# Moving the inner rows of a mixture of experts through DRAM and turning them on VectorE, with the second layer two tiles behind the first

## The chip, the cores and the metric

One core of one Trainium2 chip. The metric is the device time of one execution in microseconds. Three runs of the kernel before gave 1191.72, 1190.87 and 1191.61 us; the median is 1191.61 us.

## The reference, cut to what matters

Three stages run one after the other: a small attention, a dense two-layer network, and a mixture of experts. The change touches the last alone:

```python
N, D, E, F = 4352, 512, 8, 1024      # rows, width, experts, inner width
e_idx = np.argmax(x @ w_gate, axis=1)
for e in range(E):
    mask = e_idx == e
    h  = np.maximum(x[mask] @ w1[e], 0.0)     # first layer, 512 -> 1024
    ye = h @ w2[e]                            # second layer, 1024 -> 512
    out[mask] = gate_w[mask, None] * eom[mask, e, None] * ye
```

Everything is fp32. Each fp32 product is made of three fp32r products: both operands are split into a high part (a copy rounded to fp32r) and a low part (what is left), and hi*hi, hi*lo and lo*hi are summed.

## The kernel before, in words

The first two stages end at about 700 us of the profile and are the same in both kernels. They leave each row in a DRAM table, `buckets`, sorted by expert, and VectorE works out a small `table` of numbers from the counts: for each tile of 128 rows the bucket row at which it starts (T_ROW), the ordinal of its expert (T_ORD), whether the weights of the next expert are split during it (T_SPLIT) and those of the expert after that loaded (T_LOAD), and which of two weight slots is used. With the inputs drawn, the experts that occur get 4, 5, 13, 5, 1, 5 and 5 tiles, in this order: 38 tiles, numbered 0 to 37, with new experts at tiles 4, 9, 22, 27, 28 and 33. T_SPLIT is set at the third tile of an expert, or at its last if it has fewer: at tiles 2, 6, 11, 24, 27 and 30.

Every engine runs its own program over the tiles, in order, and waits on semaphores (`wait`, `wait_ge`). `loops` (L434) writes out the first PEEL = 3 tiles, then a hardware loop of four tiles per turn, then the tiles that may be empty, each inside an If. `entry` (L430) reads a number of the table into a register of the engine; the profile shows it as TENSOR_LOAD at L432.

TensorE (`body`, L919) does for tile t:

- `first(t)` (L877): 24 matmuls of 128x128x512 in two halves of 12, from the turned rows `xg_t` and the split weights `we` into the two banks of `h_ps`;
- `second(t-1)` (L903): 24 matmuls from `act_t` and `we` into `y_ps`;
- `transpose_hid(t)` (L893): 8 transposes (matmuls against `ident`) of `expert_hid`, the rows after the relu, into two other banks of `y_ps`. They wait for act_ready0 and act_ready1.

ScalarE (`body`, L1092): relu of the first half of tile t (L1097), high part of the next tile's rows (`rows_hi`, L1084), three table reads, if T_SPLIT the high parts of the next w1 in four pieces (L1059), the high parts of the turned inner rows (L1119, from PSUM), and if T_SPLIT those of w2. VectorE (`body`, L1506) does the relu of the second half (L1510), the low part of the next rows (L1380), low parts of the weights (L471), the gate scaling of the tile before (`put_out`, L1494), the low parts of the inner rows (L1529), and the 32x32 block transposes of the rows of tile t+2 (`turn_rows`, L1384). The rows are turned by VectorE too: SyncE loads them in four strips of 32 partitions so that block transposes are enough.

SyncE (`body`, L585) loads the rows of tile t+3 (four DMAs of 64 KB, L559, and one small one for the gates, L562), and if T_LOAD the raw w1 and w2 of the expert after next (2 MB each, L568 and L571), each as soon as its buffer has been split. GpSimd stores the finished rows with an indirect DMA (L668).

## Time and profile before

| | |
|---|---|
| median of 3 runs | 1191.61 us |
| the profiled execution | 1192.12 us |
| its span, first to last instruction | 1190.4 us (1.7 us lie around it) |
| granted TensorE clock, mean | 0.990 |
| TensorE matmul busy | 1162.4 us (98%) |
| VectorE busy | 620.1 us (52%) |
| ScalarE busy | 440.4 us (37%) |
| DMA | 91.46 MB, mean 77 GB/s |

Busy time counts tensor instructions only: an engine's table reads, branches, waits and DMA issues are not in it. Matmuls are pipelined, so a matmul of about 390 ns starts every 230 ns. The chain of waits follows the end of the span back to what released each piece; "ACTq" and "DVEq" there are the sequencers of ScalarE and VectorE, "SPq" that of SyncE.

### The profile page before, as it was taken

What the parts mean: (1) busy time and instruction counts of PE and PEld (TensorE: products, weight loads), DVE (VectorE), ACT (ScalarE), POOL (GpSimd) and SP (SyncE); (2) the same over time, 40 slices, a digit from 0 to 9 for tenths busy, and PEclk for the clock granted to TensorE, in tenths of its full rate; (3) what the DMA queues carried; (4) which work ended last, traced back from release to release, by engine and by line L of the source; (5) the groups of instructions that cost most, each with busy time, mean ns of one, the idle gap of its engine ahead of it and who ended that gap; (6) DMA issues with size and microseconds to landing.
All of it is one profiled execution on the core that took longest, in us unless ns stands there. A gap on an engine that the chain in (4) does not pass through costs nothing.

```text
span 1190.4 us, 21176 instructions
## 1 busy us (share of the span) xinstructions
PE 1162.4 (98%) x6662; PEld 916.9 (77%) x6663; DVE 620.1 (52%) x1208; ACT 440.4 (37%) x742; POOL 81.4 (7%) x96
## 2 busy tenths in 40 slices
PE   9999999999999999999999978999999999999995
PEld 7777777777777777777778966888888888878874
DVE  6675655646646546465554464654543334566331
ACT  4454444444344434444543342341412122344110
POOL 0000100001001010010010110200000000000000
PEclk9999999999999999999999988999999999999998
DMA  9211011102110111010100644335151111541111
GB/s 368 77 36 36 37 36 54 54 1 72 36 36 36 37 72 36 1 72 1 72 36 1 228 147 161 128 103 185 38 185 44 44 44 37 185 167 53 38 38 43
DMA packets 46923, 91.46 MB, mean 77 GB/s; under 512 B 10751, under 2 KB 32895, under 8 KB 42496
## 3 DMA queue, kind: packets, MB, share of 16 engines
q1 hardware_dynamic: 41088, 72.57, 18.2%
q0 software_dynamic: 5760, 17.90, 3.9%
q8 instruction: 46, 0.75, 0.3%
q14 instruction: 29, 0.24, 0.1%
HBM read 65.95 MB, written 25.55 MB: 77 GB/s over the span
## 4 chain that ended last, share of the span: by engine, by line
PE 94%; DVE 2%; issue 1%; ACT 1%; DMA 1%; POOL 0%; DVEq 0%; ACTq 0%; SPq 0%; POOLq 0%
PE y_ps L832 32%; PE h_ps L888 17%; PE y_ps L914 17%; PE h_ps L814 15%; PE y_ps L900 3%; PE a_ps L789 2%; PE h_ps L804 2%; PE a_ps L692 1%; PE a_ps L773 1%; PE a_ps L753 1%; PE b_ps L700 1%; PE b_ps L692 1%; DVE we L471 0%; PE h_ps L853 0%; PE b_ps L717 0%
## 5 line engine op out<-in xcount | busy, mean ns | idle before, releaser
L832 PE MATMUL y_ps<-w_out_hi,hid_hi 128*128 128x512 f32 x544 | 218.8, 402 | 0.0
L832 PE MATMUL y_ps<-w_out_hi,hid_lo 128*128 128x512 f32 x544 | 212.6, 391 | 0.0
L832 PE MATMUL y_ps<-w_out_lo,hid_hi 128*128 128x512 f32 x544 | 212.3, 390 | 0.0
L888 PE MATMUL h_ps<-we,xg_t_hi 128*128 (+1 forms) x608 | 197.0, 405 | 4.7 <-DVE xg_t_lo L1380 1.8
L914 PE MATMUL y_ps<-we,act_t_hi 128*128 (+1 forms) x608 | 187.9, 390 | 1.7 <-issue 1.7
L814 PE MATMUL h_ps<-att_hi,mix 128*128 128x512 f32 x512 | 185.4, 405 | 0.1
L1326 DVE SCALAR_TENSOR_TENSOR hid<-hid,h_ps 128x512 f32<-128x512 f32 (+1 forms) x144 | 94.5, 656 | 169.8 <-ACT hid L1018 168.3
L1018 ACT ACTIVATE hid<-h_ps,three 128x512 f32<-128x512 f32 (+1 forms) x144 | 95.4, 663 | 178.9 <-PE h_ps L814 155.0
L832 PEld LDWEIGHTS y_ps<-w_out_hi,hid_hi 128*128 128x128 f32 x544 | 102.1, 188 | 50.6 <-issue 30.4
L888 PEld LDWEIGHTS h_ps<-we,xg_t_hi 128*128 128x128 f32 x608 | 113.2, 191 | 31.0 <-issue 6.2
L914 PEld LDWEIGHTS y_ps<-we,act_t_hi 128*128 128x128 f32 x608 | 114.1, 188 | 26.9 <-issue 2.0
L1335 DVE TENSOR_TENSOR hid_lo<-hid,hid_hi 128x512 fp32r<-128x512 f32 (+1 forms) x144 | 94.9, 659 | 70.5 <-ACT hid_hi L1026 70.0
L1119 ACT ACTIVATE act_t_hi<-y_ps 128x512 fp32r<-128x512 f32 x76 | 41.5, 596 | 225.1 <-PE y_ps L900 223.9
L888 PE MATMUL h_ps<-we,xg_t_lo 128*128 (+1 forms) x304 | 121.5, 400 | 0.0
L832 PEld LDWEIGHTS y_ps<-w_out_hi,hid_lo 128*128 128x128 f32 x544 | 102.1, 188 | 23.6
L914 PE MATMUL y_ps<-we,act_t_lo 128*128 (+1 forms) x304 | 118.9, 391 | 0.0
L814 PEld LDWEIGHTS h_ps<-att_hi,mix 128*128 128x128 f32 x512 | 96.2, 188 | 28.9 <-issue 7.0
L832 PEld LDWEIGHTS y_ps<-w_out_lo,hid_hi 128*128 128x128 f32 x544 | 102.3, 188 | 20.3
L1026 ACT ACTIVATE hid_hi<-hid 128x512 fp32r<-128x512 f32 (+1 forms) x144 | 87.4, 607 | 66.6 <-DVE hid L1326 66.6
L814 PE MATMUL h_ps<-att_lo,mix 128*128 128x512 f32 x256 | 101.2, 395 | 0.0
L1510 DVE TENSOR_SCALAR expert_hid<-h_ps 128x512 f32<-128x512 f32 x38 | 26.0, 684 | 106.6 <-PE h_ps L888 106.6
L631 POOL DMA_INDIRECT buckets<-rows,place x34 | 34.4, 1011 | 609.5 <-DVE place L1304 601.9
(212 smaller groups left out, 1319.3 us busy)
## 6 DMA issues: line engine op xcount, KB each, us to landing
raw<-in_w SPq DMA_DIRECT2D x14, 2048.0 KB, 8.4
xg<-buckets SPq DMA_DIRECT2D x164, 64.0 KB
xb<-in_x_rows SPq DMA_DIRECT2D x8, 1024.0 KB, 4.8
x_t<-in_x_t SPq DMA_DIRECT2D x7, 1024.0 KB, 5.0
buckets<-pad_row SPq DMA_DIRECT2D x8, 774.0 KB, 8.3
w_in_raw<-in_w_in SPq DMA_DIRECT2D x4, 1024.0 KB, 12.8
raw_out<-in_w_out SPq DMA_DIRECT2D x4, 1024.0 KB, 15.0
x_t_second<-in_x_t SPq DMA_DIRECT2D x1, 1024.0 KB, 19.4
```

The costliest lines, as they stand in the source:

```text
L631: pool.indirect_dma_start(out=buckets, out_offset=bass.IndirectOffsetOnAxis(ap=place[:, t:t + 1], axis=0), in_=rows[:, t, :], in_offset=No ...
L814: i = pe.matmul(h_ps[:, j % 2, 0:cols], mix[:, m % SLOTS, g, n % GO, wp, :], (att1_hi, att1_lo)[tp][:, g, 0:cols], start=(g == 0 and k == ...
L832: i = pe.matmul(y_ps[:, t, :], (hid_hi, hid_lo)[hp][:, hid_at(b, j), t * P:(t + 1) * P], w_out_s[wp][:, j, :], start=(j == 0 and m == 0), ...
L888: i = pe.matmul(hid_ps[:, h, :], xg_t[xp][:, slot % 2, k, :], we[:, bass.ds(w_at + (wp * WPART + k * F + h * BANK), BANK)], start=(k == 0 ...
L900: i = pe.transpose(hid_t_ps[:, h, q * P:(q + 1) * P], expert_hid[:, f * P:(f + 1) * P], ident[:])
L914: i = pe.matmul(y2_ps[:, slot % 2, :], act_t[hp][:, slot % 2, f, :], we[:, bass.ds(w_at + (wp * WPART + KD * F + f * DM), DM)], start=(f = ...
L1018: act.activation(hid[:, hid_at(b, j), 0:cols], h_ps[:, j % 2, 0:cols], ACT.Relu, bias=three).then_inc(sem("relu_ready"), 1)
L1026: act.activation(hid_hi[:, hid_at(b, j), 0:cols], hid[:, hid_at(b, j), 0:cols], ACT.Copy).then_inc(sem("hid_hi_ready"), 1)
L1119: act.activation(act_t[HI][:, slot % 2, h * 4:h * 4 + 4, :].rearrange("p f t -> p (f t)"), hid_t_ps[:, h, :], ACT.Copy).then_inc(sem("act_ ...
L1326: dve.scalar_tensor_tensor(out=hid[:, hid_at(b, j), 0:cols], in0=hid[:, hid_at(b, j), 0:cols], scalar=6.0, in1=h_ps[:, j % 2, 0:cols], op0 ...
L1335: dve.tensor_tensor(hid_lo[:, hid_at(b, j), 0:cols], hid[:, hid_at(b, j), 0:cols], hid_hi[:, hid_at(b, j), 0:cols].bitcast(F32), ALU.subtr ...
L1510: dve.tensor_scalar(expert_hid[:, BANK:2 * BANK], hid_ps[:, 1, :], 0.0, None, ALU.max).then_inc(sem("act_ready1"), 1)
```

## The change

The transposes on TensorE go. After the relu, which ScalarE now does for both halves, SyncE writes a tile's 128x1024 inner rows to a DRAM buffer `hidden` (two DMAs of 256 KB) and, when these have landed, reads them back in four DMAs of 128 KB, a quarter of the columns onto 32 partitions each (`hid_mv`). VectorE turns each half with a block transpose into `act_raw`, which shares its place with the low part of `act_t`; ScalarE makes the high part from it and VectorE the low part. w2's rows are laid out on the host in the order that this gives.

`second` runs two tiles behind `first` (LAG2 = 2), and `first` takes its two banks in turn from `h_ps` and from the banks that the transposes used. SyncE no longer loads the later experts' weights: ScalarE issues those DMAs (`load_w1` one tile after T_LOAD's, `load_w2` two after). w1 is split in the tile of T_SPLIT as before, w2 in the tile after it, each at the end of ScalarE's and VectorE's body. ScalarE's body reads the table nine times per tile in place of three (thirteen where it loads a w1 and a w2, eleven where one of them). Four tiles are written out ahead of the loop in place of three. The table gets one more column (T_FIRST), one more VectorE instruction ahead of it.

```diff
+    hidden = nc.dram_tensor("hidden", [2, P, F], F32, kind="Internal").ap()
+    T_ROW, T_LIVE, T_FINAL, T_ORD, T_SPLIT, T_LOAD, T_NEXT, T_SLOT, T_OTHER, T_FIRST, T_N = range(11)
+    act_raw = at("act_raw", 147456 + 8192, [P, 2, KE, P], F32)
-    xg = at("xg", 163840, [P, RING, STRIPS, P], F32)
+    xg = at("xg", 163840, [P, 2, STRIPS, P], F32)
+    hid_mv = at("hid_mv", 163840 + 2 * STRIPS * P * 4, [P, 2, STRIPS, P], F32)
-    y2_ps, hid_t_ps, hid_ps = y_ps[:, 0:2, :], y_ps[:, 2:4, :], h_ps
+    LAG2 = 2
+    y2_ps = y_ps[:, 0:2, :]
+    hid2_banks = h_ps, y_ps[:, 2:4, :]
     N_SCATTER = CH * B + ST
     HALVES = F // BANK
-    PEEL = 3
+    PEEL = 4
...
         def load_rows(t):
-            slot = t.slot
-            wait(sp, f"out_stored{slot}", 16 * t.turn())
+            place = t.slot % 2
+            of_tile = tile_rows(t)
+            if not (t.first or is_b(t.n, 1)):
+                wait(sp, "xg_turned", t.n - 1)
...
+        def load_gate(t):
+            of_tile = tile_rows(t)
+            wait(sp, "out_ready", t.n - (RING - 1))
+            sp.dma_start(gate_s[:, t.slot, :], of_tile[:, DM:ROW]).then_inc(sem(f"gate_loaded{t.slot}"), 16)
...
         def body(t):
-            if not (isinstance(t.n, int) and t.n + RING > MT):
-                load_rows(t.plus(RING - 1))
-            load = entry(sp, t, T_LOAD)
-            with sp.If(load > 0):
-                load_expert(t.n, entry(sp, t, T_ORD, E - 3) + 2)
+            if not (isinstance(t.n, int) and t.n + 3 >= MT):
+                load_rows(t.plus(3))
+            load_gate(t)
+            place = t.slot % 2
+            if not (t.first or is_b(t.n, 1)):
+                wait(sp, "hid_moved", 16 * STRIPS * (t.n - 1))
+            for h in range(HALVES):
+                wait(sp, "act_ready", HALVES * t.n + h + 1)
+                sp.dma_start(hidden[place, :, h * BANK:h * BANK + BANK], expert_hid[:, h * BANK:h * BANK + BANK]
+                             ).then_inc(sem("hid_written"), 16)
+            wait(sp, "hid_written", 16 * HALVES * (t.n + 1))
+            wait(sp, "hid_turned", HALVES * t.n)
+            for j in range(STRIPS):
+                sp.dma_start(hid_mv[NS * j:NS * j + NS, :, :, :],
+                             hidden[place].rearrange("(s t) (h q c) -> q t h s c", t=NS, h=HALVES, c=P)[j]
+                             ).then_inc(sem("hid_moved"), 16)
...
             wait(pe, "xg_t_ready", t.n + 1)
             for h in range(HALVES):
-                wait(pe, f"act_ready{h}", t.n)
+                if not (t.first or is_b(t.n, 1)):
+                    wait(pe, "act_ready", HALVES * (t.n - 2) + h + 1)
                 for k in range(KD):
                     for m, (xp, wp) in enumerate(PRODUCTS):
-                        i = pe.matmul(hid_ps[:, h, :], xg_t[xp][:, slot % 2, k, :],
+                        i = pe.matmul(hid2_banks[slot % 2][:, h, :], xg_t[xp][:, slot % 2, k, :],
                                       we[:, bass.ds(w_at + (wp * WPART + k * F + h * BANK), BANK)],
                                       start=(k == 0 and m == 0), stop=(k == KD - 1 and m == 2))
                 i.then_inc(sem("hid2_ps"), 1)
-        def transpose_hid(t):
-            for h in range(HALVES):
-                wait(pe, f"act_ready{h}", t.n + 1)
-                wait(pe, "act_t_ready", 0 if t.first else HALVES * (t.n - 1) + h + 1)
-                for q in range(KE // HALVES):
-                    f = h * (KE // HALVES) + q
-                    i = pe.transpose(hid_t_ps[:, h, q * P:(q + 1) * P], expert_hid[:, f * P:(f + 1) * P], ident[:])
-                i.then_inc(sem("act_t_ps"), 1)
         def second(t):
             wait(pe, "w2_ready", expert + 1)
             wait(pe, "act_t_ready", HALVES * (t.n + 1))
-            wait(pe, "out_ready", t.n - 1)
+            wait(pe, "out_ready", t.n - 1 if not t.first else 0)
             for f in range(KE):
                 for m, (hp, wp) in enumerate(PRODUCTS):
             if t.first:
                 pe.wait_ge(sem("table_ready"), 1)
-            else:
-                second(t.plus(-1))
-            transpose_hid(t)
+            if not (t.first or is_b(t.n, 1)):
+                second(t.plus(-LAG2))
+        def finish(t):
+            for back in range(LAG2 - 1, -1, -1):
+                second(t.plus(-back))
         keep_warm(WARM_ROWS, y_ps[:, CH - 1, :])
-        loops(pe, body, second)
+        loops(pe, body, finish)
     @blk.scalar
...
         act.wait_ge(sem("table_ready"), 1)
+        def hidden_hi(t):
+            slot = t.slot
+            for h in range(HALVES):
+                wait(act, "hid_turned", HALVES * t.n + h + 1)
+                act.activation(act_t[HI][:, slot % 2, h * 4:h * 4 + 4, :], act_raw[:, slot % 2, h * 4:h * 4 + 4, :],
+                               ACT.Copy).then_inc(sem("act_t_hi"), 1)
+        def load_w1(e, n):
+            wait(act, "w1_ready", n)
+            act.dma_start(raw1[:], w1[bass.ds(e, 1)].rearrange("o p k f -> p (o k f)")
+                          ).then_inc(sem("raw1_loaded"), 16)
+        def load_w2(e, n):
+            wait(act, "w2_ready", n)
+            act.dma_start(raw2[:], w2[bass.ds(e, 1)].rearrange("o p j d -> p (o j d)")
+                          ).then_inc(sem("raw2_loaded"), 16)
         def body(t):
             if not t.last:
                 rows_hi(t.plus(1))
+            for h in range(HALVES):
+                wait(act, "hid2_ps", HALVES * t.n + h + 1)
+                if h == 0:
+                    wait(act, "hid_written", 16 * HALVES * t.n)
+                act.activation(expert_hid[:, h * BANK:h * BANK + BANK], hid2_banks[t.slot % 2][:, h, :], ACT.Relu
+                               ).then_inc(sem("act_ready"), 1)
+            if not t.first:
+                hidden_hi(t.plus(-1))
+            if is_b(t.n, 1):
+                load_w2(entry(act, Tile(0, MT), T_NEXT, E - 1), 1)
+            if not (t.first or is_b(t.n, 1)):
+                before_it = t.plus(-2)
+                load = entry(act, before_it, T_LOAD)
+                with act.If(load > 0):
+                    load_w2(entry(act, before_it, T_NEXT, E - 1), entry(act, before_it, T_ORD, E - 3) + 2)
+            if not t.first:
+                before_it = t.plus(-1)
+                load = entry(act, before_it, T_LOAD)
+                with act.If(load > 0):
+                    load_w1(entry(act, before_it, T_NEXT, E - 1), entry(act, before_it, T_ORD, E - 3) + 2)
+                split = entry(act, before_it, T_SPLIT)
+                n = entry(act, before_it, T_ORD, E - 1) + 1
+                other = entry(act, before_it, T_OTHER, WSLOT)
+                first_tile = entry(act, before_it, T_FIRST, MT)
+                with act.If(split > 0):
+                    if not is_b(t.n, 1):
+                        wait(act, "y2_ps", first_tile)
+                    split_hi(1, n, other)
             split = entry(act, t, T_SPLIT)
             n = entry(act, t, T_ORD, E - 1) + 1
             other = entry(act, t, T_OTHER, WSLOT)
+            with act.If(split > 0):
                 wait(act, "hid2_ps", HALVES * t.n)
                 split_hi(0, n, other)
+        loops(act, body, hidden_hi)
     @blk.vector
...
+        chain(dve.tensor_scalar(table[:, T_FIRST, 0:MT], t_start[:], 1.0, None, ALU.max))
...
-        split_lo(dve, 1, 0, 0, range(1, PIECES), "w2_ready")
...
+        def turn_hidden(t):
+            slot = t.slot
+            wait(dve, "hid_moved", 16 * STRIPS * (t.n + 1))
+            if not (t.first or is_b(t.n, 1)):
+                wait(dve, "y2_ps", t.n - 1)
+            for h in range(HALVES):
+                dve.transpose(act_raw[:, slot % 2, h * 4:h * 4 + 4, :].rearrange("p f t -> p (f t)"),
+                              hid_mv[:, h, :, :].rearrange("p s (k f) -> p k s f", f=NS)).then_inc(sem("hid_turned"), 1)
+        def hidden_lo(t):
+            slot = t.slot
+            for h in range(HALVES):
+                wait(dve, "act_t_hi", HALVES * t.n + h + 1)
+                dve.tensor_tensor(act_t[LO][:, slot % 2, h * 4:h * 4 + 4, :], act_raw[:, slot % 2, h * 4:h * 4 + 4, :],
+                                  act_t[HI][:, slot % 2, h * 4:h * 4 + 4, :].bitcast(F32), ALU.subtract
+                                  ).then_inc(sem("act_t_ready"), 1)
         def body(t):
             if not t.last:
                 rows_lo(t.plus(1))
+            if t.first:
+                split_lo(dve, 1, 0, 0, range(1, PIECES), "w2_ready")
+            if not (isinstance(t.n, int) and t.n < 3):
+                put_out(t.plus(-3))
             if not t.first:
+                turn_hidden(t.plus(-1))
             if not (isinstance(t.n, int) and t.n + 2 >= MT):
                 turn_rows(t.plus(2))
+            if not t.first:
+                hidden_lo(t.plus(-1))
+                before_it = t.plus(-1)
+                split = entry(dve, before_it, T_SPLIT)
+                with dve.If(split > 0):
+                    split_lo(dve, 1, entry(dve, before_it, T_ORD, E - 1) + 1, entry(dve, before_it, T_OTHER, WSLOT),
+                             signal="w2_ready")
+            split = entry(dve, t, T_SPLIT)
+            with dve.If(split > 0):
+                split_lo(dve, 0, entry(dve, t, T_ORD, E - 1) + 1, entry(dve, t, T_OTHER, WSLOT), signal="w1_ready")
+        def finish(t):
+            put_out(t.plus(-2))
+            turn_hidden(t)
+            hidden_lo(t)
+            put_out(t.plus(-1))
+            put_out(t)
+        loops(dve, body, finish)
...
-    give("w2", inputs["moe2_w2"].reshape(E, -1, 128, DM).transpose(0, 2, 1, 3))
+    give("w2", inputs["moe2_w2"].reshape(E, 2, 4, 4, 32, DM).transpose(0, 2, 4, 1, 3, 5).reshape(E, 128, 8, DM))
```

How the change moves instructions, as the compiled programs list them. First ScalarE, one tile of the loop, before (`we` pieces are a split of w1; the y2_ps and w2 part that follows is left out):

```order
L1097 ACTIVATE expert_hid<-h_ps 128x512 [waits act_t_ps,hid2_ps]
L1084 ACTIVATE xg_t_hi<-xg_raw 128x512 [waits hid2_ps,xg_turned]
L432 TENSOR_LOAD table
L432 ISA x3
...
L1110 COMPARE_AND_BRANCH
...
L1059 ACTIVATE we<-raw_140 128x1024
```

And one tile of the loop now, from the second half's relu on (raw_135 is raw2, raw_142 raw1; a COMPARE_AND_BRANCH passes over what follows it where the table says 0):

```order
L1135 ACTIVATE expert_hid<-h_ps 128x512 [waits hid2_ps]
L1111 ACTIVATE act_t_hi<-act_raw 128x512 [waits hid_turned] x2
L442 TENSOR_LOAD table
...
L1145 COMPARE_AND_BRANCH
...
L1123 DMA raw_135<-in_w 128x4096
...
L1150 COMPARE_AND_BRANCH
...
L1117 DMA raw_142<-in_w 128x4096
...
L1156 COMPARE_AND_BRANCH
...
L1164 COMPARE_AND_BRANCH
...
L1074 ACTIVATE we<-raw_142 128x1024
```

The split of w1 moved from behind the first relu and three table reads to the end of the body, behind both relus, the two activations that wait for VectorE's transposes, and nine table reads with four branches. Then VectorE, a tile before:

```order
L1510 TENSOR_SCALAR expert_hid<-h_ps 128x512 [waits act_t_ps,hid2_ps]
L1380 TENSOR_TENSOR xg_t_lo<-xg_raw,xg_t_hi 128x512 [waits xg_t_hi]
...
L1518 COMPARE_AND_BRANCH
...
L471 TENSOR_TENSOR we<-raw_140,we 128x1024
```

and now, the end of one:

```order
L1551 STREAM_TRANSPOSE act_raw<-hid_mv 128x512 [waits y2_ps,hid_moved]
L1551 STREAM_TRANSPOSE act_raw<-hid_mv 128x512
...
L1558 TENSOR_TENSOR act_t_lo<-act_raw,act_t_hi 128x512 [waits act_t_hi]
...
L1577 COMPARE_AND_BRANCH
...
L1581 COMPARE_AND_BRANCH
...
L481 TENSOR_TENSOR we<-raw_142,we 128x1024
```

The relu left VectorE, two transposes came, and here too w1's low parts stand last.

## Rows read from the trace of the kernel before

**Rows 1.** The page's part 1: busy time, share, instructions.
```profile
PE 1162.4 (98%) x6662; PEld 916.9 (77%) x6663; DVE 620.1 (52%) x1208; ACT 440.4 (37%) x742; POOL 81.4 (7%) x96
```
**Rows 2.** Chain of waits, a switch of experts (start us, us, what).
```profile
1023.82 0.87 PE y_ps L900 x8
1024.69 5.59 PE h_ps L888 x24
1030.28 5.47 PE y_ps L914 x24
...
1036.63 2.81 PE h_ps L888 x12
...
1040.30 0.28 ACTq L432
...
1040.91 0.28 ACTq L432
...
1048.26 1.23 DVE we L471
...
1049.82 5.86 PE h_ps L888 x24
```
**Rows 3.** Chain of waits, the first tiles.
```profile
716.64 0.20 DVE table L1487
...
723.72 8.03 PE h_ps L888 x24
```
**Rows 4.** Chain of waits, the end.
```profile
1171.03 1.73 issue
1172.76 5.74 PE y_ps L914 x24
```
**Rows 5.** Timeline of ScalarE: start us, us, instruction [idle before <-releaser].
```profile
1015.22 2.01 ACT L1059 ACTIVATE we<-raw 128x1024 f32 x2
...
1020.81 0.63 ACT L1084 ACTIVATE xg_t_hi<-xg_raw 128x512 fp32r<-128x512 f32 x1 [3.10 <-DVE xg_raw L1390]
```
**Rows 6.** Instructions on the table, 1019 to 1023 us: ns min/median/max, first and last start.
```profile
L432 ACTq TENSOR_LOAD <-table x3: 271/273/278, 1020.9 to 1022.1; - x3
```
**Rows 7.** Groups by line, 740 to 1150 us: busy us, mean ns.
```profile
L471 DVE TENSOR_TENSOR we<-raw,we 128x1024 f32 x48 | 55.5, 1219 | 7.5 <-ACT we L1059 7.5
L1503 DVE TENSOR_SCALAR yo<-y_ps,gate_s 128x512 f32<-128x512 f32 x34 | 25.2, 742 | 0.0
L1390 DVE STREAM_TRANSPOSE xg_raw<-xg 128x512 f32<-128x512 f32 x35 | 24.6, 704 | 7.1 <-DMA xg<-buckets 6.0 <-issue 1.0
L1380 DVE TENSOR_TENSOR xg_t_lo<-xg_raw,xg_t_hi 128x512 fp32r<-128x512 f32 x34 | 23.2, 684 | 0.9
L1059 ACT ACTIVATE we<-raw 128x1024 f32 x48 | 46.8, 1053 | 6.4 <-issue 6.4
L1119 ACT ACTIVATE act_t_hi<-y_ps 128x512 fp32r<-128x512 f32 x68 | 37.0, 596 | 198.4 <-PE y_ps L900 198.4
```
**Rows 8.** The page's part 6, DMA issues: KB each, us to landing.
```profile
xb<-in_x_rows SPq DMA_DIRECT2D x8, 1024.0 KB, 4.8
gate_s<-buckets SPq DMA_DIRECT2D x41, 2.0 KB, 1.8
```
**Rows 9.** Timelines of SyncE and VectorE, one tile's row loads and their use.
```profile
704.52 1.76 SPq L559 DMA_DIRECT2D xg<-buckets  x4
707.88 0.71 DVE L1390 STREAM_TRANSPOSE xg_raw<-xg 128x512 f32<-128x512 f32 x1 [1.33 <-DMA xg<-buckets]
```
**Rows 10.** Landing of the 2 MB weight loads, us min/median/max.
```profile
DMA to landing us min/median/max: 7.4/8.4/12.6
```
**Rows 11.** Busy time in stretches: us, PE, PEld, DVE, ACT, POOL, PEclk, DMA share, GB/s.
```profile
721.70:728.50 6.80, 5.90 (x15) 4.51 (x16) 2.49 (x4) 0.60 (x1) 0.00 (x0) 0.50 0.94 341
...
1047.00:1053.00 6.00, 4.75 (x26) 3.77 (x25) 6.00 (x9) 4.83 (x7) 0.97 (x1) 1.00 0.04 15
```

More of the change, by code:

```diff
@@ L1102, in body @@
             other = entry(act, t, T_OTHER, WSLOT)
-            def next_w1():
+            with act.If(split > 0):
                 wait(act, "hid2_ps", HALVES * t.n)
                 split_hi(0, n, other)
-            if not t.first:
-                with act.If(split > 0):
-                    next_w1()
-            if is_b(t.n, 1):
-                split_0 = entry(act, Tile(0, 0), T_SPLIT)
-                with act.If(split_0 > 0):
-                    split_hi(1, 1, WSLOT)
-            for h in range(HALVES):
-                wait(act, "act_t_ps", HALVES * t.n + h + 1)
-                act.activation(act_t[HI][:, slot % 2, h * 4:h * 4 + 4, :].rearrange("p f t -> p (f t)"),
-                               hid_t_ps[:, h, :], ACT.Copy).then_inc(sem("act_t_hi"), 1)
-            with act.If(split > 0):
-                if t.first:
-                    next_w1()
-                else:
-                    wait(act, "y2_ps", t.n)
-                    split_hi(1, n, other)
-        loops(act, body)
+        loops(act, body, hidden_hi)
     @blk.vector
@@ L1515, in body @@
-            n = entry(dve, t, T_ORD, E - 1) + 1
-            other = entry(dve, t, T_OTHER, WSLOT)
+            if t.first:
+                split_lo(dve, 1, 0, 0, range(1, PIECES), "w2_ready")
+            if not (isinstance(t.n, int) and t.n < 3):
+                put_out(t.plus(-3))
             if not t.first:
-                with dve.If(split > 0):
-                    split_lo(dve, 0, n, other, signal="w1_ready")
-                if is_b(t.n, 1):
-                    split_0 = entry(dve, Tile(0, 0), T_SPLIT)
-                    with dve.If(split_0 > 0):
-                        split_lo(dve, 1, 1, WSLOT, signal="w2_ready")
-                put_out(t.plus(-1))
```

70 lines of the change are left out of this document (21 added, 49 removed).

## The prediction

> **What bounds the kernel now.** I read the page's part 1 first: TensorE's matmuls are busy 98% of the span [rows 1]. So only two things can shorten the kernel: fewer matmuls, or less waiting of TensorE; and anything that makes TensorE wait lengthens it. Next I read the chain of waits over a few tiles. A tile of the expert stage is 0.87 us of transposes, 5.59 us of `first` and 5.47 us of `second`, back to back, 11.93 us in all [rows 2]. The one place with a wait in mid-stage is tile 28, the second new expert in two tiles: `first(27)` starts at 1036.63, the reads, splits and low parts follow, and `first(28)` starts 13.19 us later instead of 11.93 [rows 2]. At the start, `first(1)` takes 8.03 us in place of 5.59 [rows 3]: the granted clock is 0.50 from 721.7 to 728.5 us, the lower of the two levels (1.2 GHz), after TensorE had waited some 3 us [rows 11]. A wait of 1.2 us before tile 28 left it at 1.00 [rows 11]. The end is fixed: the last `second` ends at 1178.50 [rows 4], and 11.9 us of gating, store and closing follow to 1190.4; 1.7 us more lie around the span.
>
> **If the copies cost nothing.** The new order of TensorE is first(0), first(1), first(2), second(0), first(3), second(1) and so on, with no transposes. The table is ready at 716.84 [rows 3], 0.2 us later with its new instruction. Then the rows of tile 1 are turned (0.70), rounded (0.63) and their low part taken (0.69) [rows 7], which with the passing of semaphores gives a start of first(1) at 719.3. second(0) waits for the first copy: relu at 719.7, SyncE's row loads first, writes to 724.0, reads to 728.6 (below), turn, high and low part to 731.8, against the end of first(2) at 730.5: a wait of 1.4 us. From 719.3 there are 37 firsts and 38 seconds: 37 x 5.59 + 38 x 5.47 + 1.4 = 416.1 us, end at 1135.4, which is 43.1 us before 1178.50. 33.1 us of these are 38 x 0.87 of transposes; the rest are the waits at the start, at tile 28 and at the end (1.73 us, [rows 4]), and the slow first(1). That would be 1149.0 us against the profiled 1192.1.
>
> **The copies.** With `first(t)` starting at 0, the second relu begins at 5.9 and ends at 6.5. The page has no such write. Its bounds are 1.8 us (2 KB) and 4.8 us (1 MB) [rows 8]; I take 2.5 us for 256 KB, nearer the small one. For the reads the nearest row is a tile's row loads, the same 512-byte pieces and half the bytes: 1.76 us of issuing, used 3.4 us after the first issue [rows 9]. So 3.4 us is the lower bound, 3.4 plus what 256 KB more add by the weight loads (2 MB in 8.4, [rows 10]) makes 4.4; I take 4.3. The rows are there at 13.5. VectorE turns them after `put_out` of its next tile, ScalarE comes to them at 11.06 + 6.4 = 17.5 in its own order, the low part is done by 19, and `second(t)` starts at 27.7. So there are 8 us of spare, and the copies cost nothing in a plain tile. VectorE loses a relu and gets two turns of 0.70 [rows 7]; this too lies beside TensorE.
>
> **What is late next: ScalarE's reads of the table.** A read costs 0.61 us from start to start (1040.30 and 1040.91, [rows 2]), busy nowhere. And it can't run ahead of an activation that waits: at 1020.81 `rows_hi` began after 3.10 us of waiting [rows 5], and the three reads behind it began at 1020.9, not before [rows 6]. Now nine reads with four branches, 5.9 us, stand behind the two activations that wait for VectorE's turns. The Trainium skill speaks against this ("Perfetto Trace Analysis", section "DVE / Act Engine Instruction"): an activation that waits is pushed to a wait queue, and the sequencer goes on. By that rule the reads would run during the wait and the sum would stay near 1149 us; the trace, with 1020.9 behind 1020.81, does not agree.
>
> In a plain tile ScalarE goes: relu at 5.9, high parts at 6.4 and 6.9, reads to 12.8, then `rows_hi` of the tile after next. That with its low part (1.3 us) is due at 2 x 11.06 = 22.1: spare 8.0. When ScalarE is late the loop is: high and low part of rows (1.2), put_out (0.75), two turns (1.3), reads (5.9) = 9.2 us, so a plain tile gives back 1.9.
>
> A switch of experts, from a full spare, with start of the T_SPLIT tile at 0: reads end at 12.8; four pieces of w1 at 0.95 (two take 2.01, [rows 5]), VectorE's four at 1.14 (1.22 each, overlapping, [rows 7]) end at 18.5. Next tile: low part, put_out and turns to 21.1; eight reads, a DMA and branches 5.8, to 27.0; w2's pieces, VectorE's end at 32.7. Third tile: low part of rows at 33.3, due 33.2; put_out and turns to 35.3; eleven reads and a DMA 7.6, to 42.9; rows 1.3, to 44.2, due 44.2. So a switch eats the whole spare of 8. The next one finds what plain tiles gave back: 1.9 after four tiles, 3.8 after five. Waits of TensorE: at tile 6, 8.0 - 1.9 = 6.1; at 11, 4.2; at 2, where the spare isn't full yet, between 0 and 6, I take 3; at 24 none (nine plain tiles ahead); at 30 about 1, after the long wait of tile 28. Sum **14.3 us**.
>
> Tile 28 is the costly one. Its w1 is split in tile 27, three tiles after the switch of 24. ScalarE leaves tile 26 at 42.9; rows, put_out and turns 3.3, to 46.2; reads to 52.1; the pieces until VectorE's last, 5.8, to 57.9. Due 44.2: **13.7 us**, in place of the 1.3 before. The clock falls in such a wait: one `first` at the low level, 8.03 - 5.59 = **2.4 us**. Shorter waits may lower it too, but there TensorE's lost time runs while ScalarE catches up; I count 0, at most 3 x 2.4.
>
> The weight loads now come from ScalarE while SyncE copies. The spare of 8 hides that but for second(1); between 0 and 12.6 - 8.4 = 4.2 [rows 10], I take **2 us**. The If and loop ends cost as before. SyncE issues eleven DMAs a tile, about 5 us with its reads, and GpSimd's store is unchanged: hidden.
>
> Sum: 1149.0 + 14.3 + 13.7 + 2.4 + 2 = 1181.4 against the profiled 1192.1; the median lies 0.5 lower, so I predict **1181 us**. Bounds of the forecast: each read 0.53 instead of 0.61 gives some 10 us less, the branches twice as dear 6 us more.
>
> **Rivals.**
>
> *The cover holds.* Reads overlap with the activations, or run faster than 0.61 us. Then only tile 28 waits, 3 to 6 us, and the sum is 1149 to 1160. For it: TensorE's own reads cost nothing in the loop. Against it: [rows 2, 5, 6]. Chance 0.20.
>
> *Given back.* The small terms all fall on the dear side: branches 6 us more, second(1) and its like 2 more, one more `first` at the low level 2.4: 1191.4, and with it 1189 to 1194, no difference that a measurement can tell (for this kernel that is within 0.2%, 2.4 us). Chance 0.10.
>
> *Slower, through the copies.* The place is SyncE's reads of `hidden`. ScalarE issues w1 and w2, 2 MB each, right behind its high parts, when the copies of a tile are under way. If these stand behind a whole load, they come 8.4 to 12.6 us later [rows 10]; above 8 us of spare every load costs TensorE time, and in the late tiles of a switch all of it. Eleven loads at about 3 us: 1181 + 33 = 1214. It decides from copies that land 8 us late. Against it: the median is 8.4, just at the spare, and the DMA share is 0.04 between loads [rows 11]. Chance 0.23. By the Trainium skill ("DMA: Bandwidth & Descriptors", section "Queues, rings and completion order") each DMA engine takes turns between the queue rows of SyncE and ScalarE, packet by packet, so that the copies would share and not stand behind; that would make this rival some 5 us; no row here shows both queues at once.
>
> That the transposes are not gone is excluded: the compiled order has none.
>
> **How the numbers follow.** Forecast, 1165 to 1189 us: 0.47. Cover holds: 0.20. Given back: 0.10. Slower: 0.23. The range leaves out the lower part of the second case and the upper part of the last: 1157 to 1201 us. Faster by over 0.2%: 0.47 + 0.20 = 0.67; within 0.2%: 0.10; slower: 0.23. The likeliest case has its own range, 1165 to 1189.
>
> **What would show it.** Right: no L900; the plain tiles 11.06 us apart, from tile 14 to 24 without a wait; nine ScalarE reads per tile at 0.61 us, after the activation of L1111; a wait of TensorE of 12 to 15 us before first(28) that ends with VectorE's L481, and a granted clock of 0.50 behind it; waits of 1 to 6 us at the starts of `first` at tiles 4 to 14, released by the low part of the rows. Wrong: no such waits (the cover holds), or waits before `second` released by the low part of the inner rows whose chain leads to a DMA from `hidden` (the slower rival).

## The result and the profile after

| | before | after |
|---|---|---|
| median, us | 1191.66 (4 runs beside the other's) | 1208.48 (1207.43 to 1210.71, 4 runs) |
| ratio | | 1.0145, 95% [1.0127, 1.0163] |
| profiled execution, its span | 1192.12, 1190.4 | 1207.43, 1205.7 |
| granted TensorE clock, mean | 0.990 | 0.975 |

The changed kernel is slower by 1.45%; 1181 was forecast, with a range to 1201. Its page answers to [rows 1]: TensorE has 304 operations less and waits more. The queues of part 3 are q1 (SyncE, with the copies) and q10 (ScalarE, the weight loads).

```profile
PE 1142.7 (95%) x6358; PEld 893.1 (74%) x6359; DVE 636.8 (53%) x1247; ACT 463.8 (38%) x780; POOL 76.9 (6%) x96
...
q1 hardware_dynamic: 91360, 89.35, 23.4%
q10 hardware_dynamic: 1584, 23.07, 5.1%
```

A plain tile, in the chain of waits (start us, us, what), answers to [rows 2] without its 0.87 of transposes: 11.07 us.

```profile
937.38 5.60 PE h_ps L910 x24
942.97 5.47 PE y_ps L926 x24
```

What TensorE waited for, from 700 us on (us in total, times, longest): L910 is `first`, L926 `second`, L1418 the low part of the rows, L481 that of the weights, L1558 that of the inner rows.

```profile
PE h_ps L910 <- DVE we L481: 14.4, 1, 14.4
PE h_ps L910 <- DVE xg_t_lo L1418: 13.9, 6, 3.7
PE y_ps L910 <- DVE xg_t_lo L1418: 12.4, 6, 3.1
PE y_ps L926 <- DVE act_t_lo L1558: 4.3, 1, 4.3
```

The first row is tile 28. The next two are 1.6 us before first(0), the start (3.3 us before first(1); the kernel before waited 3.4 us there, ahead of its transposes) and 23.1 us in ten waits at the switches (by the starts of the matmuls, each some 0.15 us more than in the rows): before first(4), (5), (6) 3.7, 1.8, 0.9; (8), (9) 3.0, 2.8; (13), (14) 1.4, 3.8; (27) 2.2; (32), (33) 1.6, 1.9. The fourth is second(1).

ScalarE in tile 24, where w1 is split, which answers to [rows 5, 6]: first the chain of waits (L1551 is VectorE's turn of the inner rows, L442 a table read), then the timeline (L1111 is the high part of the inner rows, L1074 that of the weights).

```profile
1010.08 1.31 DVE act_raw L1551 x2
1011.49 0.28 ACTq L442
...
1013.06 0.28 ACTq L442
```

```profile
1010.82 1.23 ACT L1111 ACTIVATE act_t_hi<-act_raw 128x512 fp32r<-128x512 f32 x2 [0.80 <-DVE act_raw L1551]
1017.93 3.91 ACT L1074 ACTIVATE we<-raw 128x1024 f32 x4 [5.89 <-PE y_ps L910]
```

ScalarE stood idle until VectorE's first turn was done (1010.82), then did two activations; the second began at about 1011.4, and only then, at 1011.49, began the nine reads, one every 0.61 us. With their four branches they last until 1017.93, where w1's pieces start: 6.44 us. The timeline names TensorE as what ended that idle time, but the chain shows the reads.

The chain where the copies meet a weight load. First for second(1), then for first(28); L607 is SyncE's issue of a read.

```profile
721.68 2.32 DMA hidden<-expert_hid
...
731.02 9.67 DMA hidden<-expert_hid
...
742.75 2.76 DMA hid_mv<-hidden
...
1042.13 0.68 SPq L607
1042.85 9.44 DMA hid_mv<-hidden
...
1053.07 1.07 ACT act_t_hi L1111 x2
...
1061.05 1.05 ACT we L1074
...
1066.29 7.59 PE h_ps L910 x24
```

The second of a tile's two writes takes 2.32 us to landing without a load and 9.67 beside the w2 load issued at 731.03; the last of the four reads takes 2.76 without and 9.44 beside another load. Behind the read of 1042.85 come turn, high parts, 6.9 us more of reads and branches, the pieces of w1, and first(28).

The clock, in stretches (us, PE, PEld, DVE, ACT, POOL busy, PEclk, DMA share, GB/s): first(4) behind a wait of 3.7 us, a stretch without waits, and first(28).

```profile
759.78:766.88 7.10, 7.10 (x24) 5.66 (x25) 3.46 (x6) 1.22 (x2) 0.97 (x1) 0.78 0.63 161
796.00:802.00 6.00, 6.00 (x27) 4.87 (x26) 3.54 (x6) 1.31 (x3) 0.97 (x1) 1.00 0.52 176
...
1066.29:1072.50 6.21, 6.21 (x19) 4.99 (x20) 2.20 (x5) 0.60 (x1) 0.97 (x1) 0.69 0.11 42
```

A mean of 0.78 or 0.69 is part of the stretch at 2.4 and part at 1.2 GHz. Behind eight waits (2.2 to 14.5 us long) the next 24 matmuls took 7.1 to 8.4 us in place of 5.6 or 5.5; added up, 16.5 us. Behind the waits of 1.9 us and less they took 5.7.

So TensorE's time goes like this, against 1134.4 us, where it would end from first(1)'s start at 719.38 without a wait (37 x 5.60 + 38 x 5.47). It ended at 1194.86, 60.4 later: tile 28 14.5, switches 23.1, second(1) 4.4, second(37) 1.25, slow blocks 16.5, and 0.7 of small change (0.5 of it the 0.1 behind each of five short waits).

That says where TensorE stood or ran slowly, not what made the kernel late. The chain of waits says this: from 717 us to first(14) it holds no instruction of TensorE, only ScalarE, VectorE, SyncE and the copies. Pieces of it (the first two copies stand above; L1099 is the high part of the rows, here in two plain tiles in a row):

```profile
832.45 9.04 DMA hid_mv<-hidden
...
849.10 0.64 ACT xg_t_hi L1099
...
859.00 0.64 ACT xg_t_hi L1099
...
890.26 8.47 PE h_ps L910 x24
```

From first(14) on it runs through TensorE but for 998 to 1066 us, ahead of first(28), 1107 to 1127, ahead of first(33), and the end. So of the eight slow blocks only first(14) and first(28) stand in the chain, with 2.7 and 1.8 us. While the other six ran slowly, ScalarE was late anyway.

### The profile page after: what moved, and what is told of

Read it like the earlier page. It is cut to its first block, busy times and chain, and to the rows that moved or that the text cites. A ratio compares the mean times of both kernels' runs of the same rounds, so it can differ in the third digit from the quotient of the medians.

```text
span 1205.7 us, 21805 instructions
## 1 busy us (share of the span) xinstructions
PE 1142.7 (95%) x6358; PEld 893.1 (74%) x6359; DVE 636.8 (53%) x1247; ACT 463.8 (38%) x780; POOL 76.9 (6%) x96
## 3 DMA queue, kind: packets, MB, share of 16 engines
q10 hardware_dynamic: 1584, 23.07, 5.1%
## 4 chain that ended last, share of the span: by engine, by line
PE 74%; ACTq 6%; issue 5%; DVE 5%; DMA 3%; ACT 3%; SPq 1%; DVEq 1%; POOL 0%; POOLq 0%
PE y_ps L853 32%; PE h_ps L835 15%; PE y_ps L926 9%; ACTq L442 5%; PE y_ps L910 5%; PE h_ps L910 5%; PE a_ps L810 2%; PE h_ps L825 2%; DMA hid_mv<-hidden 2%; DMA hidden<-expert_hid 1%; ACT we L1074 1%; DVE we L481 1%; DVE act_raw L1551 1%; ACT act_t_hi L1111 1%; PE a_ps L713 1%
## 5 line engine op out<-in xcount | busy, mean ns | idle before, releaser
L926 PE MATMUL y_ps<-we,act_t_hi 128*128 (+1 forms) x608 | 189.1, 392 | 5.4 <-DVE act_t_lo L1558 4.3
L926 PEld LDWEIGHTS y_ps<-we,act_t_hi 128*128 128x128 f32 x608 | 114.8, 189 | 31.2 <-issue 6.2
L910 PE MATMUL h_ps<-we,xg_t_hi 128*128 (+1 forms) x304 | 102.8, 421 | 28.3 <-DVE we L481 14.4
L926 PE MATMUL y_ps<-we,act_t_lo 128*128 (+1 forms) x304 | 119.4, 393 | 0.0
L910 PE MATMUL y_ps<-we,xg_t_hi 128*128 x304 | 100.4, 412 | 12.4 <-DVE xg_t_lo L1418 12.4
L1418 DVE TENSOR_TENSOR xg_t_lo<-xg_raw,xg_t_hi 128x512 fp32r<-128x512 f32 x39 | 26.9, 689 | 151.5 <-ACT xg_t_hi L1099 151.5
L481 DVE TENSOR_TENSOR we<-raw,we 128x1024 f32 (+1 forms) x55 | 63.9, 1219 | 68.4 <-ACT we L1074 68.3
L1099 ACT ACTIVATE xg_t_hi<-xg_raw 128x512 fp32r<-128x512 f32 x39 | 24.5, 627 | 182.4 <-issue 139.6
L910 PEld LDWEIGHTS h_ps<-we,xg_t_hi 128*128 128x128 f32 x304 | 60.9, 203 | 45.4 <-issue 31.2
```

Source lines behind the costliest of these rows:

```text
L481: ins = eng.tensor_tensor(we[:, bass.ds(w_at + piece(w, i, LO), PIECE)], raw[:, i * PIECE:(i + 1) * PIECE], we[:, bass.ds(w_at + piece(w, ...
L910: i = pe.matmul(hid2_banks[slot % 2][:, h, :], xg_t[xp][:, slot % 2, k, :], we[:, bass.ds(w_at + (wp * WPART + k * F + h * BANK), BANK)], ...
L926: i = pe.matmul(y2_ps[:, slot % 2, :], act_t[hp][:, slot % 2, f, :], we[:, bass.ds(w_at + (wp * WPART + KD * F + f * DM), DM)], start=(f = ...
L1099: act.activation(xg_t[HI][:, slot % 2, :, :], xg_raw[:, slot % 2, :, :], ACT.Copy).then_inc(sem("xg_t_hi"), 1)
L1418: dve.tensor_tensor(xg_t[LO][:, slot % 2, :, :], xg_raw[:, slot % 2, :, :], xg_t[HI][:, slot % 2, :, :].bitcast(F32), ALU.subtract).then_i ...
```

## The experiments

Theory A: ScalarE's reads, in order behind its waiting activations, set the waits at the switches, and the place of w1's split that of tile 28. Theory B: the copies that stand behind weight loads set them. Theory C: VectorE's work. Each kernel is the changed one with an edit, unless said otherwise.

| kernel | median, us | ratio to before, 95% |
|---|---|---|
| few_reads | 1190.43 | 0.9988 [0.996, 1.0015] |
| more_reads | 1257.32 | 1.0563 [1.0535, 1.0592] |
| small_loads | 1195.56 | 1.0041 [1.0022, 1.006] |
| w1_first | 1188.69 | 0.998 [0.9965, 0.9995] |
| few_w1_first | 1177.11 | 0.9854 [0.981, 0.9898] |
| small_packets | 1210.92 | 1.0166 [1.0146, 1.0186] |
| few_w1_packets | 1172.82 | 0.9865 [0.9809, 0.992] |
| few_w1_small_loads | 1152.63 | 0.9683 [0.9663, 0.9702] |
| few_w1_sp_loads | 1257.72 | 1.0557 [1.054, 1.0575] |
| before_reads | 1192.32 | 1.0007 [0.9997, 1.0016] |
| w2_load_first | 1190.69 | 0.9991 [0.9981, 1.0001] |
| w2_load_first_packets | 1194.17 | 1.0019 [1.0009, 1.0029] |
| gap_loads | 1201.4 | 1.0076 [1.0058, 1.0093] |
| gap_loads_packets | 1204.09 | 1.0109 [1.0095, 1.0122] |

### Fewer reads, more reads

```diff
                 split = entry(act, before_it, T_SPLIT)
-                n = entry(act, before_it, T_ORD, E - 1) + 1
-                other = entry(act, before_it, T_OTHER, WSLOT)
-                first_tile = entry(act, before_it, T_FIRST, MT)
                 with act.If(split > 0):
+                    n = entry(act, before_it, T_ORD, E - 1) + 1
+                    other = entry(act, before_it, T_OTHER, WSLOT)
+                    first_tile = entry(act, before_it, T_FIRST, MT)
```

and the same for the `n` and `other` of w1's split.

> The changed kernel with five of ScalarE's nine table reads per tile moved into the branch that needs them, so that a plain tile has four reads and a tile of a switch still has all. Theory A (the in-order reads behind ScalarE's waiting activations set the waits of TensorE): a plain tile gives back 3.0 us more (5 x 0.61), so most of the 23.1 us of waits before first(4) to first(14), 27, 32 and 33 go, the wait before first(28) falls from 14.5 to about 10, and with the fewer low-clock stretches behind them the time is some 30 us less: about 1178 us (1168 to 1190). Theory B (the copies stand behind the weight loads and set the waits): the loads and copies are as before, so no change, 1205 to 1210 us. Theory C (VectorE's turns and splits set them): also no change.

Measured 1190.43, 18.0 us less: just past the dear end of theory A's range. Of the waits of L910 for L1418, eight of twelve are left, and tile 28 has 10.8 in place of 14.4:

```profile
PE y_ps L910 <- DVE xg_t_lo L1418: 13.5, 4, 5.4
PE h_ps L910 <- DVE we L481: 10.8, 1, 10.8
PE h_ps L910 <- DVE xg_t_lo L1418: 5.5, 4, 2.0
```

Theories B and C expected no change and can't stand alone. But before first(9), at 821.84, there now is a wait of 5.6 us, longer than the changed kernel's 2.8, and its chain goes back over w2's and w1's pieces to a write that took 6.47 us: B has a share.

```profile
780.97 6.47 DMA hidden<-expert_hid
```

```diff
+            for _ in range(4):
+                entry(act, t, T_ORD, E - 1)
```

> The changed kernel with four more table reads per tile at the end of ScalarE's tile, whose values nobody uses. Theory A: ScalarE's loop when it is late grows by 2.4 us (4 x 0.61), from about 9.8 to 12.2 us, over TensorE's 11.07 us a tile; so nothing is given back and every tile waits once the spare is gone: some 60 to 100 us more, about 1290 us (1260 to 1320). Theories B and C (copies behind loads; VectorE): up to 5 us more, 1208 to 1214.

Measured 1257.32: 48.8 us more, ten times what B and C allowed and a little under A's range, presumably since the reads take effect only in tiles where ScalarE is late. Now 22 waits for the rows' low part:

```profile
PE y_ps L910 <- DVE xg_t_lo L1420: 31.4, 14, 3.9
PE h_ps L910 <- DVE xg_t_lo L1420: 20.1, 8, 4.8
PE h_ps L910 <- DVE we L481: 16.6, 1, 16.6
```

The same was done to the kernel before, with six reads:

> The kernel before with six unused table reads (3.7 us) at the end of ScalarE's tile, which makes as many as the changed kernel has. Theory A (a read costs only where ScalarE has no slack): in the kernel before ScalarE stands between first and transposes of every tile, waiting for TensorE some 5 us, so the reads run while first runs: plain tiles stay at 11.93 us, and only the chain at tile 28 grows by up to 3.7 us: 1192 to 1197 us. If a read costs TensorE time anywhere: 38 x 3.7 us more.

Measured 1192.32 against 1191.53, ratio 1.0007 [0.9997, 1.0016]: as theory A has it. In its chain a plain tile is what it was in [rows 2]:

```profile
941.75 5.59 PE h_ps L888 x24
947.34 5.47 PE y_ps L914 x24
952.81 0.87 PE y_ps L900 x8
```

Six reads cost nothing that can be measured where ScalarE has time to spare; in the changed kernel, where it has none at a switch, four cost 48.8 us.

### The place of w1's split

ScalarE's `body` then begins like this (VectorE's does its four pieces right behind `rows_lo`):

```diff
                 rows_hi(t.plus(1))
+            if not t.first:
+                load = entry(act, t.plus(-1), T_LOAD)
+                with act.If(load > 0):
+                    load_w1(...)
+            split = entry(act, t, T_SPLIT)
+            n = entry(act, t, T_ORD, E - 1) + 1
+            other = entry(act, t, T_OTHER, WSLOT)
+            with act.If(split > 0):
+                wait(act, "hid2_ps", HALVES * t.n)
+                split_hi(0, n, other)
```

> The changed kernel with the split of w1 (with its reads and the issue of the w1 load) moved from the end of a tile to right behind the rows' high part on ScalarE, and right behind the rows' low part on VectorE; the work and the nine reads are the same. Theory A with its place (at tile 28 the pieces of w1 stand behind the hidden rows' high parts and eight other reads): the wait of 14.5 us before first(28) and its low-clock stretch go, and the waits at the other switches become a little shorter: about 1186 us (1178 to 1196). If it is the sum of ScalarE's work and not its place that makes first(28) wait: a change of under 4 us, 1204 to 1210. Theory B: no change.

Measured 1188.69, 19.8 us less, with work and reads the same: the place decides at tile 28. The edit moves the pieces of both engines, so which engine's place matters was not separated. A wait of 3.8 us is left there, and waits before `second` are new:

```profile
PE y_ps L926 <- DVE act_t_lo L1559: 15.6, 6, 5.2
...
PE h_ps L910 <- DVE we L481: 3.8, 1, 3.8
```

> The changed kernel with both edits: five reads moved into the branches that need them, and w1's load and split right behind the rows' high and low part. Theory A (reads and the place of w1's split): the two gains of 18 and 20 us add, 1170 us (1166 to 1176). Theory B (what is left is copies that stand behind weight loads: waits before second and first of 5 us each in the two runs apart): the gains overlap, since each run already had new waits behind the copies, 1176 to 1184 us.

Measured 1177.11. The gains of 18.0 and 19.8 overlap (31.4 together), as B had it, though its runs went from 1168.74 to 1180.35. With few_w1_packets, from which its interval can't tell it, it is the fastest kernel here that computes everything, and beats the kernel before by 1.5%. No wait for rows or weights at a switch is over 1.1 us; what is left stands before `second`. Its chain before second(13):

```profile
866.25 7.75 DMA hidden<-expert_hid
...
885.80 7.59 DMA hid_mv<-hidden
```

### The weight loads

```diff
-            act.dma_start(raw1[:], w1[...].rearrange("o p k f -> p (o k f)")
+            act.dma_start(raw1[:, 0:512], w1[...].rearrange("o p k f -> p (o k f)")[:, 0:512]
```

and the same for w2.

> The changed kernel with ScalarE's weight loads cut to 512 of 4096 columns (256 KB in place of 2 MB); the rest of each expert's weights is what the buffer held, so the output leaves out most of the new weights. Theory A: only the wait before second(1) (4.4 us and 1.7 us of low clock) and a few us of the chain of first(28) hang on the loads: about 1200 us (1196 to 1206). Theory B (copies stand behind the loads and set the waits at the switches): the waits at tiles 4 to 14 and most of that of 28 go: 1160 to 1185 us.

Measured 1195.56, 12.9 us less: just below A's range and far above B's (the profiled run was the slowest of the five, 1203.25). Tile 28 waits as long as before, so its wait is not the copies' doing, though its chain above passes through a read of 9.44 us: ScalarE is as late without it.

```profile
PE h_ps L910 <- DVE we L481: 14.5, 1, 14.5
```

> The kernel with fewer reads and w1 first, and ScalarE's weight loads cut to 512 of 4096 columns; the output leaves out most of the new weights. It shows what is left when the copies never meet a load. Theory B: only the start (3.3 us), tile 28 (0 to 3 us) and the end wait, 1150 to 1158 us. Theory A alone (loads don't matter): no less than the kernel with two edits.

Measured 1152.63; the profiled run took 1150.61 and has almost no wait but that of the start. Its page's TensorE row shows how much TensorE ran slowly before: the same 6358 operations in 16.3 us less busy time than in the changed kernel. 14.9 of these are the slow blocks; of the eight only first(1) is left, 1.6 us.

```profile
PE 1126.4 (98%) x6358; PEld 883.9 (77%) x6359; DVE 644.9 (56%) x1247; ACT 465.5 (41%) x780; POOL 77.0 (7%) x96
```

Taking the loads' bytes away is worth 12.9 us in the changed kernel and 24.5 behind a quick ScalarE: how much a cause is worth depends on the others.

> The kernel with fewer reads and w1 first, and its weight loads issued by SyncE, whole, right behind the reads of the tile's hidden rows, in place of by ScalarE. Bytes are the same. The load then starts when the tile's copies are done and ends some 4 us after the next tile's writes are due (reads done at 13.5 of a tile's start, load to 22, writes at 17.6), so the copies are late by 4 us and not 7 to 9, inside the spare of 8: the waits before second(2), second(6), second(13), second(29) go, 1158 to 1168 us. If SyncE's own issuing (about 8 of 11 us a tile, now with two or three reads more) is what decides, it gets no better: 1175 to 1195 us.

Measured 1257.72, 80.6 us more than with ScalarE's loads: my first theory fell, and the second was too mild. SyncE's own timeline in one tile of a switch (start us, us, issue): in 15 us it does nothing but issue, read and wait for its write.

```profile
771.02 0.36 SPq L612 DMA_DIRECT2D hidden<-expert_hid  x1
775.14 2.59 SPq L617 DMA_DIRECT2D hid_mv<-hidden  x4
780.92 0.36 SPq L572 DMA_DIRECT2D raw<-in_w  x1
...
785.54 0.83 SPq L612 DMA_DIRECT2D hidden<-expert_hid  x2
```

Behind a load in its own queue a write takes up to 5.9 us to landing in place of 2.3, and in plain tiles SyncE's writes follow each other in 11.1 to 11.3 us (959.1, 970.4, 981.5), no less than TensorE's 11.07, so little is given back. Another place in SyncE's order was not tried.

> The kernel with fewer reads and w1 first, and the w2 load too issued at the top of ScalarE's tile (behind the rows' high part), some 4 us earlier in the tile, before the tile's write of hidden rows instead of beside it. If a copy that meets a load late in its run loses less than one that meets it at its start, the waits before second(2), (6), (13) and (29), 12.2 us with their slow clock 7.7 us, shrink: 1165 to 1172 us. If the copies lose about a load's time wherever the two meet, it is the same as before the move: 1174 to 1180 us.

Measured 1190.69, 13.6 us more; neither expectation. A ScalarE that isn't late gets to the top of its tile while the last tile's reads are under way, and then one tile's copies meet both loads. Chain before second(12):

```profile
867.38 7.93 DMA hidden<-expert_hid
...
877.29 9.97 DMA hid_mv<-hidden
```

The next kernel adds to it, ahead of each load:

```diff
+                    wait(act, "hid_moved", 16 * STRIPS * t.n)
```

> The kernel with fewer reads and both w1's split and both loads at the top of ScalarE's tile, and before each load a wait until the hidden rows of the tile before have landed. Bytes and instructions are the same but for that wait. If the meeting in time decides: the load runs in the gap between one tile's reads (landed 2.4 us into the next) and that tile's write (due at 6.5), the write is late by some 4 us, inside the spare of 8, and the waits before second(0), (3), (12) and (28) of 20.6 us with 8.6 us of slow clock go but for the first: 1160 to 1168 us. If the amount of transfers decides, or the wait costs ScalarE as much as it saves: 1185 to 1195 us, as the kernel without the wait (1190.7).

Measured 1201.4, 10.7 us more again; neither expectation. The wait holds up everything behind it on ScalarE. In its timeline ScalarE's relu, which starts the next copy, comes behind 11.5 and 10.1 us without work; the load is issued 1.2 and 2.1 us before that relu, when the copies have landed; ten waits for the inner rows' low part are left, 23.0 us, in place of seven, 22.1.

```profile
756.70 0.35 ACTq L1117 DMA_DIRECT2D raw<-in_w  x1
757.86 1.09 ACT L1155 ACTIVATE expert_hid<-y_ps 128x512 f32<-128x512 f32 x2 [11.52 <-issue]
...
774.91 1.08 ACT L1155 ACTIVATE expert_hid<-h_ps 128x512 f32<-128x512 f32 x2 [10.10 <-PE y_ps L910]
```

So whether a load put between the copies would be free is not shown: the test paid more than it could save.

### The size of the pieces

Each 2 MB load becomes two DMAs of every second 512 columns, so its pieces are 2 KB and not 16 KB (q10 has 11616 packets in place of 1584):

```diff
+            for h in range(2):
+                act.dma_start(raw1[:].rearrange("p (k f) -> p k f", k=KD)[:, :, h * BANK:h * BANK + BANK],
+                              w1[...].rearrange("o p k f -> p (o k) f")[:, :, h * BANK:h * BANK + BANK]
```

> The changed kernel with each weight load cut into two DMAs of every second 512-column block, so that its pieces are 2 KB in place of 16 KB; same bytes, one more DMA issue per load. If the DMA engines take turns between ScalarE's and SyncE's queue piece by piece (theory P), a write of the hidden rows (8 pieces of 2 KB per engine and half) beside a load lands in about 5 us in place of 9.7, and the wait before second(1) goes: 1198 to 1204 us. If a load that is under way goes first as a whole (theory Q), nothing changes: 1207 to 1212 us.

> The changed kernel with all three edits: fewer reads in a plain tile, w1 first, and weight loads in pieces of 2 KB. Theory P: the writes share with a load and only the reads (64 pieces of 512 bytes per engine) still take as long as a load; the waits behind the copies are halved against the kernel with two edits: 1158 to 1170 us. Theory Q: as the kernel with two edits.

> The same kernel with the weight loads in pieces of 2 KB. The first kernel with such pieces gained nothing (1210.9 against 1208.5), the second perhaps 4 us (1172.8 against 1177.1, the intervals overlap): here it tells whether the pieces matter at all. If they share with the writes: 3 to 8 us below the kernel with 16 KB pieces; if not: equal within 2 us.

> The same with the weight loads in pieces of 2 KB. In three pairs so far they were 2 us slower, 4 us faster (not resolved) and 3.5 us slower; I expect within 4 us of the kernel with 16 KB pieces, either way.

Measured, in this order, 1210.92, 1172.82, 1194.17 and 1204.09. Against their partners with 16 KB pieces: 2.4 more, 4.3 less (the intervals of the two overlap almost wholly), 3.5 more, 2.7 more. The first fits theory Q's range; the second can't be told from its partner, which is theory Q too; the third fits neither of its two; the fourth is as expected. There is no gain in time to be had by the size.

Yet the queues do take turns piece by piece. The DMA view counts the packets, each one piece, of the two queues. First the changed kernel from 733 to 738 us, with the w2 load and the write of 9.67 us both under way; then few_w1_first from 867 to 871, with a load and the write of 7.75 us; then small_packets from 733 to 737, where the four reads of a tile were issued from 733.19 on, behind the load:

```profile
q10 hardware_dynamic: 99, 1.62, 85.8%
q1 hardware_dynamic: 99, 0.20, 10.4%
...
q10 hardware_dynamic: 85, 1.39, 100.9%
q1 hardware_dynamic: 85, 0.00, 1.2%
...
q10 hardware_dynamic: 699, 1.40, 102.1%
```

In the first two the turns are one for one: 99 pieces of 2 KB against 99 of 16 KB, then 85 against 85. The 85 are not the write's: they are pieces of 16 bytes of the gates' load, 2 KB in all, which SyncE issues ahead of the write, and the write stands behind them in the same queue. In the third the reads got no piece at all for 4 us, while the load had 699; the last of them took 6.88 us. The write before them had landed in 3.05 us, most of it ahead of the load's first piece, and the wait before second(1) fell from 4.3 to 0.9 us, as theory P has it; but the waits for the rows' low part grew from 26.3 to 34.6 us. So theory P is right on the turns of pieces that are under way, and not on a read that is issued behind a load. What holds such a read up isn't shown.

## Why the prediction was wrong

**Right.** No transposes; plain tiles 11.07 us apart (11.06) and no wait from tile 15 to 26; first(1) at 719.38 (719.3); the reads in order behind the activations of L1111; a wait of 14.5 us (13.7) before first(28), ended by L481, the clock low behind it. The sum if the cover holds, 1149.0, was nearly met: few_w1_small_loads took 1150.61 in its profiled run. That is luck in part: the sum had 1.4 for second(0) and 1.1 of closing too much, and 1.6 for first(1)'s slow block too little. By the Trainium skill ("Perfetto Trace Analysis", section "DVE / Act Engine Instruction") an activation that waits is pushed to a wait queue, and the sequencer is ready for the next instruction. The trace disagrees again, as [rows 5, 6] did, with a first read at 1011.49 behind the activation at 1011.4. more_reads gives the price of four reads more, 48.8 us.

**The step that failed: "The spare of 8 hides that but for second(1)", 2 us, and the length of ScalarE's loop beside it.** Without a wait first(14) would start at 857.8 us. The forecast has 16.7 us of delay before it (1.4 for second(0), 2 for contention, 3, 6.1 and 4.2 at the switches); it started at 890.26, 32.4 late. These 15.7 us are the largest error. I counted the spare of 8 twice, once for ScalarE's reads and once for the copies. The chain of waits up to first(14) has both: a write that took 9.67 us for 2.32, a read that took 9.04 for some 2.8, and ScalarE's tiles between them. These were longer than forecast, too: the reads with branches took 6.44 and not 5.9, and a plain tile of a late ScalarE 9.90 (849.10 to 859.00) and not 9.2, so that it gives back 1.2 us and not 1.9. The experiments show both causes, by the start of first(14) in the profiled runs: 880.72 with fewer reads, 881.30 with small loads, 883.70 with w1 first, 876.80 with few_w1_first, and 860.46 with all three edits. The gains of reads and loads overlap, so 15.7 us can't be divided between them.

The waits at the switches show the same tile by tile, 23.1 for 14.3 us: the first switch 6.4 for 3, the second 5.8 for 6.1, tile 11's 5.2 for 4.2, tile 24's 2.2 for none, tile 30's 3.5 for 1. few_reads, which changes only the reads, takes away some of them and not all (21.6 us of L910's waits for the rows at the switches become 14.9).

**From first(14) on.** Up to first(28) TensorE lost 21.1 us for 13.7: the wait of 14.5, and in front of it 2.2 of wait and 1.6 of slow block at first(27), and 2.7 of slow block at first(14). From there to the end it lost 6.9 for 3.4: waits of 3.5 for 1 at tile 30's switch, 1.25 before second(37), a slow block of 1.8 for 2.4.

**The clock, 2.4 us.** I counted one slow `first`; there were eight slow blocks, 16.5 us. [rows 3, 11] had shown the fall behind 3 us of waiting, and four of my own waits (3, 6.1, 4.2, 13.7) and that before first(1) were of that size. But this is not 14.1 us of time. I had argued that "TensorE's lost time runs while ScalarE catches up", and by the chain that holds for six of the eight: first(9) starts at 828.18, released by a chain through ScalarE's reads and pieces of w2, while the slow first(8) was over at 819.92. In the chain stand 2.7 and 1.8 us, 2.1 over the term. No run holds the clock up, so this rests on the chain alone.

**The rival "slower, through the copies"** had the right row (a copy lands in 9.0 to 9.7 us beside a load) and the right sign: the chain of second(1)'s wait of 4.4 us leads to copies from and to `hidden`. Its price, 33 us, did not come: small_loads shows 12.9, and 24.5 once ScalarE is quick. second(0) did not wait (0 for 1.4).

Summed: 15.7 up to first(14), 7.4 up to first(28), 3.5 behind it, 0.4 of start and block lengths, less 1.1 of a shorter closing: 26, from 1181.4 to 1207.4. Without waits TensorE would have ended 44 us earlier than before (1134.4 for 1178.50), 33.1 of them transposes; 60.4 came back.

What stays open: the share of reads, branches and late copies in each wait, and what holds up a read that is issued behind a load. By the Trainium skill ("DMA: Bandwidth & Descriptors", section "Queues, rings and completion order") an engine drains a whole packet of one queue, 9 to 17 descriptors as a rule, before it turns to the other. The trace doesn't agree: with 99 pieces of each queue, and 85 of each, the turns were of single pieces.

## What to carry to other kernels

Busy time doesn't show an engine's table reads: count them (0.61 us each) in the loop that the engine runs when it is late, and put those that only a branch needs inside it. When a change takes work off the bounding engine by lengthening the chain behind it, the spare of that chain must hold at its worst stretch, here three tiles of a switch in a row, and it can be spent only once: add up all that draws on it in the same tiles. A wait of TensorE of over some 2 us can be followed by 1.5 to 2.8 us of slow clock (in the other kernels a few of 2.1 to 3.5 us were followed by none), but that costs time only where the chain comes back to TensorE behind it. Look at what stands ahead of a copy in its queue: here 2 KB in pieces of 16 bytes took as many turns beside a load as 2 MB in pieces of 16 KB. Moving a load or adding a wait on an in-order queue moves everything behind it: three such moves here cost 10.7 to 80.6 us.

## What the runs showed that I had not expected

- Copies (writes of 256 KB, reads of 128 KB) that met a 2 MB load from another queue in the chain took 6.5 to 10 us to landing in place of 2.3 to 2.8, both the writes and the reads.
- The runs of one kernel spread more than those of another: the kernel before 1189.73 to 1193.02 in 18 runs, few_reads 1184.6 to 1198.55 in 8. A profile is one of these runs, so its waits need not add up to the median's difference.
- The clock fell behind eight separate waits, and for six of them it cost no time by the chain. What decides whether it falls behind a wait of 2 to 3.5 us isn't shown.
